# A batch's small state read with token blocks outermost, in a fused attention and two-layer expert kernel

## The chip, the cores and the metric

The kernel runs on one core of one Trainium2 chip. The metric is the device time in microseconds of one execution; lower is better. A number given for a kernel is the median of several executions. One more execution of it was recorded by the hardware profiler, and every duration below is from that record.

## What is computed

Three stages follow each other. The change lies in the attention; the rest is what TensorE spends most of its time on.

```python
# attention, B=4, H=8, S=512 tokens, 32 state rows, D=64
scores  = x @ state.T / sqrt(D);  a  = softmax(scores)   # over the 32 state rows
xread   = a @ state
scores2 = state @ x.T / sqrt(D);  a2 = softmax(scores2)  # over the 512 tokens
sread   = a2 @ x                                         # "read of the state": 32 x 64 a head
# rows of xread and sread, heads side by side: 2176 tokens x 512
h = t @ w_in;  g = h * tanh(softplus(h));  y = g @ w_out # 512 -> 2048 -> 512
# top-1 of 8 experts by the cosine to expert_emb, then
out = gate * (relu(y @ w1[e]) @ w2[e])                   # 512 -> 1024 -> 512
```

All is float32. Large products are made as three products of split operands: each operand is a rounded high part (`WH`, `Ah`, `gh`) and a low rest (`WL`, `Al`, `gl`).

## The kernel before, in words

The engines' programs are written out by hand, one instruction stream for each of TensorE (PE), ScalarE (ACT), VectorE (DVE), GpSimd and the DMA issuer, and they meet at counting semaphores. Nothing is reordered by a scheduler: an instruction that waits holds up all that stands behind it in its engine's stream.

The 2048 hidden columns are taken in 8 pieces of 256 for each batch c (0 to 3), numbered v = 8c + p. For each piece PE computes `H(v)` (line 599: 12 products into PSUM banks 0 and 1, or 6 and 7), ACT and DVE compute the activation together in six passes of 1024 columns (`mish_t`, `mish_w`, `mish_b`, `mish_c`, `mish_hi` on ACT, lines 1032 to 1064; `mish_q`, `mish_e`, `mish_r`, `mish_g`, `mish_lo` on DVE, lines 1500 to 1526), and PE computes `Y(v)` (line 647: 24 products that add to banks 2 to 5). PE's order is H two pieces ahead of Y: H(6), Y(4), H(7), Y(5), H(8), and so on. `H(v)` waits until `mish_q(v-1)` has read its piece out of PSUM, and the first H of a batch c waits for both parts of A, the softmax weights of that batch: `A_hi(c)` on ACT (line 1000, copies `AF` to `Ah`) and `A_lo(c)` on DVE (line 1453, the rest into `Al`).

Beside this runs the attention of the next batch. `M(c, nb)` (line 535) multiplies the state into w_in, and `M_hi` (ACT, line 971) and `M_lo` (DVE, line 1361) take its result out of banks 6 and 7. `score(c)` (line 506) writes banks 6 and 7, `scores_out` (ACT, line 982) takes the scores to `SC`; from batch 1 on it first waits until `SC` was read by the transpose of the batch before (`e2d_rdy`).

The state's read of a batch, `sread(b)` (line 551), is the part that the change is about. `soft_5(b)` (DVE, line 1435) adds 1e-9 to the two sums of each partition, takes their reciprocals, and transposes `SC` into `E2D`. `sread(b)` then makes 128 small products of 32x32 by 32x64: for each of two head groups g and 16 token blocks t, four heads j, each on its own row block and column block of PE's array. The trace has two matmul records and two weight-load records for each of them. For b = 0 all 128 stand between H(6) and Y(4) (line 807); for the others 64 stand at one place and 64 at a later one (`ahead`, `behind`). Before the change b = 0 and 1 run g outermost, with column block j and both groups in bank 6; b = 2 and 3 run t outermost, with column block j^g and bank 6+g. Because column block j^1 puts the heads of group 1 at other partitions, the reciprocals of group 1 are there taken in four instructions of 32 partitions (line 1448). PE waits at `sread(0)` for `e2d_rdy` and for `scores_out(1)` (`sc_e` 4). `sread_scale(b)` (DVE, line 1462) multiplies the result by the reciprocals, `sread_turned(b)` (PE, line 562) transposes it after Y(4), and `sread_out(b)` (ACT, line 1008, four copies for b < 2, or line 1011, two copies) places it in `sh`, which M(1, 0) waits for.

The order around the change is this, u being the piece whose activation is under way. DVE for u = 5: mish_e, mish_r, soft_1(1), mish_g, mish_q(6), mish_lo, sread_scale(0), o_rest(5), soft_sum/soft_3/soft_4(1). DVE for u = 6: mish_e, mish_r, M_lo(1,0), mish_g, mish_q(7), A_lo(1), mish_lo, o_rest(6). ACT for u = 6: mish_b, o_split(6), sread_out(0), mish_t(7), M_hi(1,0), mish_c, mish_w(7), A_hi(1), mish_hi. (`o_split` and `o_rest` split a block of w_out, lines 976 and 1375.)

Of the kernel before, what the change touches and what calls it, by code (L numbers as in the profile page):

```python
# [41 lines left out]
def build(nc, x, state, w_in, w_out, emb, tau, w1, w2, out):  # L42
# [10 lines left out]
    HG = H // 4  # L53
# [30 lines left out]
    def upto(u, e=1):  # L84

        return e + 1 if u == 0 else u + 2
# [26 lines left out]
    with ExitStack() as ctx:  # L113
# [168 lines left out]


        def sr_bank(b, g):
            return 6 if b < 2 else 6 + g

        def sh_upto(b):
            return (4, 8, 10, 12)[b]

        def bv_upto(b):  # L290
            return (2, 4, 10, 16)[b]

        def y_bank(t):
            return 1 if first(t) else 2
# [202 lines left out]
        def _(pe):  # L497
# [41 lines left out]
            def sread(b, part):  # L539
                pe.wait_ge(e2d_rdy, b + 1)  # L540
                if b > 1:
                    pe.wait_ge(m_lo, NB * b + 2)
                elif b == 1:
                    pe.wait_ge(rt_e, ST)
                else:
                    pe.wait_ge(sc_e, 4)
                order = [(g, t) for g in range(HG) for t in range(16)] if b < 2 else [(g, t) for t in range(16) for g in range(HG)]
                for g, t in order[part]:
                    for j in range(4):
                        q = j if b < 2 else j ^ g  # L550
                        mm = pe.matmul(PS[32 * q:32 * q + 32, sr_bank(b, g), D * g:D * g + D], E2D[b][32 * j:32 * j + 32, g, 32 * t:32 * t + 32],  # L551
                                       X2[b % 2][t // 8][32 * j:32 * j + 32, g, t % 8, :],
                                       start=(t == 0), stop=(t == 15))
                if part.stop is None:
                    mm.then_inc(sr_mm, 1)
# [245 lines left out]
            for v in range(B * PC):  # L801
# [3 lines left out]
                if c == 0:  # L805
                    if p == 4:
                        sread(0, whole)
# [123 lines left out]
            with pe.Fori(0, less4) as i:  # L931
                t = (i, 3)
# [16 lines left out]
        def _(act):  # L949
# [16 lines left out]
            def M_hi(c, nb, bank=6):  # L966
                k = NB * c + nb
                act.wait_ge(m_mm, k + 1)
                if k >= NM:
                    act.wait_ge(h_mm, upto(2 * (k - NM) + 1))  # L970
                a.activation(WH[:, k % NM].rearrange("p (g n) -> p g n", g=HG), PS[:, bank:bank + 2, :], ACT.Copy).then_inc(m_hi, 1)

            def o_split(k):
                r = RING["o", k]
                act.wait_ge(in_w[r % NSTAGE], 16 * (r // NSTAGE + 1))
                a.activation(WH[:, 8 + k], raw[:, r % NSTAGE], ACT.Copy).then_inc(o_hi, 1)
# [17 lines left out]
            def A_hi(b, gs=range(HG)):  # L994
                act.wait_ge(af_rdy, HG * b + gs[-1] + 1)
                if b == 1 or b == 2:
                    act.wait_ge(sr_mm, b)
                if b >= 2:
                    act.wait_ge(h_mm, upto((b - 1) * PC - 1))
                a.activation(Ah[:, b % 2, gs[0]:gs[-1] + 1], AF[:, gs[0]:gs[-1] + 1], ACT.Copy).then_inc(a_hi, len(gs))  # L1000

            def sread_out(b):
                act.wait_ge(sh_t, b + 1)
                ps = PS[0:D, 6 if b == 1 else 7, 0:HG * P].rearrange("p (g q r n) -> p g q r n", g=HG, q=2, r=2)
                for h in range(2):
                    if b < 2:
                        for g in range(HG):
                            a.activation(sh[D * h:D * h + D, 2 * g:2 * g + 2, NS * b:NS * b + NS], ps[:, g, :, h if g == 0 else 1 - h, :],
                                         ACT.Copy).then_inc(sh_e, 1)
                    else:  # L1010
                        a.activation(sh[D * h:D * h + D, :, NS * b:NS * b + NS].rearrange("p (g q) n -> p g q n", g=HG), ps[:, :, :, h, :],
                                     ACT.Copy).then_inc(sh_e, 1)
# [42 lines left out]
            def mish_c(u, es=slice(0, 2)):  # L1055
                act.wait_ge(e_rdy, upto(u, es.stop - 1))
                a.activation(ww[:, u % 2, es], ww[:, u % 2, es], ACT.Square, bias=cst[:, 0:1]).then_inc(s_rdy, 1)  # L1057
# [116 lines left out]
            for u in range(1, PC):  # L1174
                mish_b(u)
                if u == 5:
                    scores_out(1)
                if u == 6:
                    o_split(6)
                    sread_out(0)  # L1180
                if u < PC - 1:
                    mish_t(u + 1)
                if u == 2:
                    M_hi(0, 2, 0)
                if u == 3:
                    o_split(3)
                if u == 4:
                    M_hi(0, 3)
                if u == 6:
                    M_hi(1, 0)  # L1190
                mish_c(u)
                if u == PC - 1:
                    o_split(7)
                    break
                mish_w(u + 1)
                if u == 6:
                    A_hi(1)
                mish_hi(u)
                if u == 1:
                    o_split(2)  # L1200
                if u == 3:
                    exp_2(0)
                if u == 4:
                    o_split(4)
                    o_split(5)
                if u == 5:
                    exp_1(1)
# [147 lines left out]
        def _(dve):  # L1355
            v = nc.vector

            def M_lo(c, nb, bank=6):
                k = NB * c + nb
                dve.wait_ge(m_hi, k + 1)  # L1360
                v.tensor_tensor(WL[:, k % NM].rearrange("p (g n) -> p g n", g=HG), PS[:, bank:bank + 2, :],
                                WH[:, k % NM].rearrange("p (g n) -> p g n", g=HG).bitcast(F32), ALU.subtract).then_inc(m_lo, 1)
# [72 lines left out]
            def soft_5(b):  # L1435
                dve.wait_ge(s2_x, 2 * b + 2)
                if b == 1:
                    dve.wait_ge(h_mm, upto(PC - 1))
                v.tensor_scalar(r2[:, b % 2, 2, :], r2[:, b % 2, 2, :], 1e-9, None, ALU.add).then_inc(bv, 1)
                if b < 2:  # L1440
                    dve.wait_ge(bv, bv_upto(b) - 1)
                    v.reciprocal(r2[:, b % 2, 3, :], r2[:, b % 2, 2, :]).then_inc(bv, 1)
                else:
                    dve.wait_ge(bv, bv_upto(b) - 5)
                    v.reciprocal(r2[:, b % 2, 3, 0:1], r2[:, b % 2, 2, 0:1]).then_inc(bv, 1)
                    for j in range(4):
                        q = j ^ 1
                        v.reciprocal(r2[32 * q:32 * q + 32, b % 2, 3, 1:2], r2[32 * j:32 * j + 32, b % 2, 2, 1:2]).then_inc(bv, 1)
                v.transpose(E2D[b][:], SC[:]).then_inc(e2d_rdy, 1)
# [66 lines left out]
            def mish_g(u, es=slice(0, 2)):  # L1516
                dve.wait_ge(qr_rdy, upto(u, es.stop - 1))
                dve.wait_ge(s_rdy, upto(u, es.stop - 1))
                to = qq[:, u % 2, es] if SEQ[u][0] == "m" else gz[SEQ[u][2]][:]
                v.scalar_tensor_tensor(out=to, in0=ww[:, u % 2, es], scalar=0.75, in1=qq[:, u % 2, es],  # L1520
                                       op0=ALU.add, op1=ALU.mult).then_inc(g_rdy, 1)
# [173 lines left out]
            for u in range(1, PC):  # L1695
                mish_e(u)
                mish_r(u)
                if u == 5:
                    soft_1(1)
                if u == 2:  # L1700
                    M_lo(0, 2, 0)
                if u == 4:
                    M_lo(0, 3)
                if u == 6:
                    M_lo(1, 0)
                mish_g(u)
                if u == PC - 1:
                    o_rest(7)
                    break
                mish_q(u + 1)  # L1710
                if u == 6:
                    A_lo(1)
                mish_lo(u)
                if u == 5:
                    sread_scale(0)
                if u == 1:
                    o_rest(2)
                    soft_2(0)
                if u > 2:
                    o_rest(u)  # L1720
                if u == 2:
                    turn_x(1, 0)
                    turn_x(1, 1)
                if u == 3:
                    turn_x(1, 2)
                    turn_x(1, 3)
                if u == 4:
                    soft_5(0)
                if u == 5:
                    soft_sum(1)  # L1730
                    soft_3(1)
                    soft_4(1)
# [231 lines left out]
```

## Time and profile before

| | |
|---|---|
| median of 3 executions | 662.65 us (662.56 to 662.71) |
| profiled execution | 663.51 us, of which the span from first to last instruction is 661.7 us |
| PE busy in the span | 644.3 us, 97% |
| DVE, ACT busy | 441.0 us (67%), 389.7 us (59%) |
| granted TensorE clock | full to within the last 6 us of the span; mean 0.997 |

A view of the trace called the chain of waits follows the work that ended last back to what released each step. The timeline lists instructions of an engine in order of time; "[0.36 <-ACT WH L971]" behind one says that the engine was idle for 0.36 us before it and that line 971 of ACT ended that. "issue" is time in which an engine waited for nothing that the record shows. An instruction may start some 0.1 us before the one before it on its engine has ended.

### The profile page before, as it was taken

The numbers are of one execution on the slowest core, as the hardware profiler recorded it, in microseconds if no ns is written. First come the engines' busy times: TensorE is split into PE (matmuls) and PEld (weight loads), VectorE is DVE, ScalarE is ACT, GpSimd is POOL, SyncE is SP. The second block draws the span as 40 slices with busy tenths as digits, with TensorE's granted clock in tenths as the row PEclk, the third lists the DMA queues.
The fourth block names the chain that finished last, engine by engine and source line by source line (L and its number), as shares of the span: only waits on it lengthen the run. The fifth ranks groups of instructions, "written<-read, shape, count | busy, mean of one in ns | idle before, by whom it ended". The sixth has DMA issues, their size and how long they took to land.

```text
span 661.7 us, 12475 instructions
## 1 busy us (share of the span) xinstructions
PE 644.3 (97%) x4186; PEld 496.8 (75%) x4187; DVE 441.0 (67%) x697; ACT 389.7 (59%) x505; POOL 52.4 (8%) x76
## 2 busy tenths in 40 slices
PE   7899899999999999999999999999999999999996
PEld 5677677677776777776668888788888888888884
DVE  6899999998788689775669668644521631271271
ACT  2898778796668786786877472533421631261260
POOL 2000000000300002100002131100100100100101
PEclk9999999999999999999999999999999999999998
DMA  8913457100533001434000723744511541163140
GB/s 230 273 40 116 174 139 211 64 2 1 152 106 128 1 0 30 166 124 131 0 1 34 263 75 114 274 169 143 191 32 48 175 147 48 48 213 120 48 159 6
DMA packets 35351, 72.73 MB, mean 110 GB/s; under 512 B 5699, under 2 KB 5699, under 8 KB 35312
## 3 DMA queue, kind: packets, MB, share of 16 engines
q1 hardware_dynamic: 27728, 56.93, 26.7%
q0 software_dynamic: 3040, 9.13, 3.5%
q10 hardware_dynamic: 4544, 6.14, 3.0%
q8 instruction: 26, 0.43, 0.3%
q14 instruction: 13, 0.11, 0.1%
HBM read 60.92 MB, written 12.16 MB: 110 GB/s over the span
## 4 chain that ended last, share of the span: by engine, by line
PE 75%; DVE 12%; ACT 6%; issue 3%; DMA 3%; SPq 1%; POOL 0%; ACTq 0%; DVEq 0%; POOLq 0%
PE PS L647 20%; PE PS L754 16%; PE PS L783 16%; PE PS L599 8%; PE PS L763 2%; PE PS L628 2%; PE PS L551 2%; PE PS L535 2%; PE PS L668 1%; DVE ww L1508 1%; ACT ww L1057 1%; DVE qq L1520 1%; PE PS L506 1%; DVE qq L1503 1%; PE PS L735 1%
## 5 line engine op out<-in xcount | busy, mean ns | idle before, releaser
L647 PE MATMUL PS<-WH,gh 128*128 128x512 f32 x256 | 104.0, 406 | 1.4 <-DVE gl L1526 1.3
L647 PE MATMUL PS<-WH,gl 128*128 128x512 f32 x256 | 101.0, 394 | 0.0
L647 PE MATMUL PS<-WL,gh 128*128 128x512 f32 x256 | 100.9, 394 | 0.0
L1157 ACT ACTIVATE hh<-PS 128x512 fp32r<-128x512 f32 x40 | 21.9, 595 | 91.3 <-PE PS L763 88.8
L1602 DVE TENSOR_TENSOR WL<-raw,WH 128x1024 f32 (+1 forms) x48 | 56.0, 1220 | 19.9 <-ACT WH L1137 19.9
L783 PE MATMUL PS<-WH,hh 128*128 (+1 forms) x160 | 65.3, 408 | 0.0
L647 PEld LDWEIGHTS PS<-WH,gh 128*128 128x128 f32 x256 | 48.2, 188 | 19.9 <-issue 6.5
L783 PE MATMUL PS<-WH,hl 128*128 (+1 forms) x160 | 63.1, 394 | 0.0
L783 PE MATMUL PS<-WL,hh 128*128 (+1 forms) x160 | 62.9, 393 | 0.0
L1621 DVE TENSOR_SCALAR osb<-PS,gid 128x512 f32<-128x512 f32 x21 | 15.7, 749 | 66.9 <-PE PS L783 66.9
L1137 ACT ACTIVATE WH<-raw 128x1024 f32 (+1 forms) x48 | 47.6, 1054 | 21.0 <-issue 13.5
L647 PEld LDWEIGHTS PS<-WH,gl 128*128 128x128 f32 x256 | 48.2, 188 | 11.3
L1057 ACT ACTIVATE ww<-ww,cst 128x1024 f32<-128x1024 f32 (+1 forms) x35 | 39.4, 1125 | 28.5 <-DVE ww L1508 28.5
L647 PEld LDWEIGHTS PS<-WL,gh 128*128 128x128 f32 x256 | 48.3, 189 | 10.0
L1503 DVE SCALAR_TENSOR_TENSOR qq<-ww,PS 128x1024 f32<-128x1024 f32 (+1 forms) x35 | 41.4, 1181 | 20.8 <-ACT ww L1045 20.8
L1149 ACT ACTIVATE hsb<-PS 128x512 f32<-128x512 f32 x42 | 24.3, 593 | 51.8 <-PE PS L754 44.3
L1508 DVE SCALAR_TENSOR_TENSOR ww<-ww,rr 128x1024 f32<-128x1024 f32 (+1 forms) x35 | 41.5, 1187 | 15.5 <-ACT rr L1053 15.4
L754 PE MATMUL PS<-WH,yh 128*128 (+1 forms) x168 | 47.7, 405 | 1.3 <-DVE yl L1607 1.3
L754 PE MATMUL PS<-WH,yl 128*128 (+1 forms) x168 | 46.0, 395 | 0.0
L754 PE MATMUL PS<-WL,yh 128*128 (+1 forms) x168 | 45.9, 395 | 0.0
L1607 DVE TENSOR_TENSOR yl<-PS,yh 128x512 fp32r<-128x512 f32 x21 | 14.4, 688 | 47.2 <-ACT yh L1143 47.1
L1520 DVE SCALAR_TENSOR_TENSOR qq<-ww,qq 128x1024 f32<-128x1024 f32 (+1 forms) x33 | 39.3, 1190 | 7.7 <-ACT ww L1057 7.4
(276 smaller groups left out, 1245.9 us busy)
## 6 DMA issues: line engine op xcount, KB each, us to landing
raw<-in_w SPq DMA_DIRECT2D x48, 512.0 KB, 4.6
raw<-in_w_in SPq DMA_DIRECT2D x36, 512.0 KB, 4.9
yg<-by_expert ACTq DMA_DIRECT2D x22, 260.0 KB
raw<-in_w_out SPq DMA_DIRECT2D x8, 512.0 KB, 6.0
by_expert<-junk SPq DMA_DIRECT2D x1, 2080.0 KB, 9.8
wr<-in_w_in SPq DMA_DIRECT2D x4, 512.0 KB, 10.2
x_0a<-in_x SPq DMA_DIRECT2D x8, 128.0 KB, 4.4
x_0b<-in_x SPq DMA_DIRECT2D x8, 128.0 KB, 5.3
```

Source lines behind the costliest of these rows:

```text
L599: mm = pe.matmul(PS[:, h_bank(v) + e, :], w[:, (NB * c + p // 2) % NM, o:o + P], a[:, c % 2, g, :], start=(i == 0 and g == 0), stop=(i == ...
L647: mm = pe.matmul(PS[:, 2 + t, :], a[:, v % 2, e, t * P:t * P + P], w[:, 8 + p, e * 512:e * 512 + 512], start=(p == 0 and e == 0 and i == 0 ...
L754: mm = pe.matmul(PS[:, j, :], a[:, k, :], w[:, bass.ds(slot + k, 1), j * 512:j * 512 + 512].rearrange("p o n -> p (o n)"), start=(i == 0 a ...
L783: mm = pe.matmul(PS[:, o_bank(t, end), :], a[:, m, :], w[:, bass.ds(slot + (KT + m // 2), 1), (m % 2) * 512:(m % 2) * 512 + 512].rearrange ...
L1057: a.activation(ww[:, u % 2, es], ww[:, u % 2, es], ACT.Square, bias=cst[:, 0:1]).then_inc(s_rdy, 1)
L1137: a.activation(WH[:, bass.ds(slot + b, 1), :].rearrange("p o n -> p (o n)"), raw[:, b % NSTAGE], ACT.Copy).then_inc(w_hi, 1)
L1149: a.activation(hsb[:, j * 512:j * 512 + 512], PS[:, j, :], ACT.Relu).then_inc(hs_rdy, 1)
L1157: a.activation(hidden(end)[0][:, 4 * j:4 * j + 4, :], PS[:, 3 + j, :].rearrange("p (k m) -> p k m", k=4), ACT.Copy).then_inc(hh_rdy, 1)
L1503: v.scalar_tensor_tensor(out=qq[:, u % 2, es], in0=ww[:, u % 2, es], scalar=4.0, in1=PS[:, bank + es.start:bank + es.stop, :], op0=ALU.sub ...
L1508: v.scalar_tensor_tensor(out=ww[:, u % 2, es], in0=ww[:, u % 2, es], scalar=4.0, in1=rr[:, es], op0=ALU.add, op1=ALU.mult).then_inc(e_rdy, 1)
L1520: v.scalar_tensor_tensor(out=to, in0=ww[:, u % 2, es], scalar=0.75, in1=qq[:, u % 2, es], op0=ALU.add, op1=ALU.mult).then_inc(g_rdy, 1)
L1602: v.tensor_tensor(WL[:, bass.ds(slot + b, 1), :].rearrange("p o n -> p (o n)"), raw[:, b % NSTAGE], WH[:, bass.ds(slot + b, 1), :].rearran ...
```

## The change

For batch 0 the state's read is done as for batches 2 and 3: t outermost, column block j^g, bank 6+g, reciprocals in five instructions, two copies out. Batch 1 stays as it was. Semaphore counts follow. On ACT `sread_out(0)` moves ahead of `o_split(6)`, and `A_hi(1)` moves from behind `mish_w(7)` to ahead of `mish_c(6)`. On DVE `A_lo(1)` moves from behind `mish_q(7)` to ahead of `mish_g(6)`, and `sread_scale(0)` from behind `mish_lo(5)` to ahead of `mish_q(6)`.

```diff
--- before.py
+++ after.py
@@ -282,13 +282,13 @@
 
 
         def sr_bank(b, g):
-            return 6 if b < 2 else 6 + g
+            return 6 if b == 1 else 6 + g
 
         def sh_upto(b):
-            return (4, 8, 10, 12)[b]
+            return (2, 6, 8, 10)[b]
 
         def bv_upto(b):
-            return (2, 4, 10, 16)[b]
+            return (6, 8, 14, 20)[b]
 
         def y_bank(t):
             return 1 if first(t) else 2
@@ -544,10 +544,10 @@
                     pe.wait_ge(rt_e, ST)
                 else:
                     pe.wait_ge(sc_e, 4)
-                order = [(g, t) for g in range(HG) for t in range(16)] if b < 2 else [(g, t) for t in range(16) for g in range(HG)]
+                order = [(g, t) for g in range(HG) for t in range(16)] if b == 1 else [(g, t) for t in range(16) for g in range(HG)]
                 for g, t in order[part]:
                     for j in range(4):
-                        q = j if b < 2 else j ^ g
+                        q = j if b == 1 else j ^ g
                         mm = pe.matmul(PS[32 * q:32 * q + 32, sr_bank(b, g), D * g:D * g + D], E2D[b][32 * j:32 * j + 32, g, 32 * t:32 * t + 32],
                                        X2[b % 2][t // 8][32 * j:32 * j + 32, g, t % 8, :],
                                        start=(t == 0), stop=(t == 15))
@@ -1003,7 +1003,7 @@
                 act.wait_ge(sh_t, b + 1)
                 ps = PS[0:D, 6 if b == 1 else 7, 0:HG * P].rearrange("p (g q r n) -> p g q r n", g=HG, q=2, r=2)
                 for h in range(2):
-                    if b < 2:
+                    if b == 1:
                         for g in range(HG):
                             a.activation(sh[D * h:D * h + D, 2 * g:2 * g + 2, NS * b:NS * b + NS], ps[:, g, :, h if g == 0 else 1 - h, :],
                                          ACT.Copy).then_inc(sh_e, 1)
@@ -1176,8 +1176,8 @@
                 if u == 5:
                     scores_out(1)
                 if u == 6:
+                    sread_out(0)
                     o_split(6)
-                    sread_out(0)
                 if u < PC - 1:
                     mish_t(u + 1)
                 if u == 2:
@@ -1188,13 +1188,12 @@
                     M_hi(0, 3)
                 if u == 6:
                     M_hi(1, 0)
+                    A_hi(1)
                 mish_c(u)
                 if u == PC - 1:
                     o_split(7)
                     break
                 mish_w(u + 1)
-                if u == 6:
-                    A_hi(1)
                 mish_hi(u)
                 if u == 1:
                     o_split(2)
@@ -1437,7 +1436,7 @@
                 if b == 1:
                     dve.wait_ge(h_mm, upto(PC - 1))
                 v.tensor_scalar(r2[:, b % 2, 2, :], r2[:, b % 2, 2, :], 1e-9, None, ALU.add).then_inc(bv, 1)
-                if b < 2:
+                if b == 1:
                     dve.wait_ge(bv, bv_upto(b) - 1)
                     v.reciprocal(r2[:, b % 2, 3, :], r2[:, b % 2, 2, :]).then_inc(bv, 1)
                 else:
@@ -1703,16 +1702,15 @@
                     M_lo(0, 3)
                 if u == 6:
                     M_lo(1, 0)
+                    A_lo(1)
                 mish_g(u)
                 if u == PC - 1:
                     o_rest(7)
                     break
-                mish_q(u + 1)
-                if u == 6:
-                    A_lo(1)
-                mish_lo(u)
                 if u == 5:
                     sread_scale(0)
+                mish_q(u + 1)
+                mish_lo(u)
                 if u == 1:
                     o_rest(2)
                     soft_2(0)
```

## Rows read from the trace of the kernel before

**Rows 1.** The page: the chain that ended last, by engine.

```profile
PE 75%; DVE 12%; ACT 6%; issue 3%; DMA 3%; SPq 1%; POOL 0%; ACTq 0%; DVEq 0%; POOLq 0%
```

**Rows 2.** The chain of waits, 60 to 100 us: start us, us, what.

```profile
75.67 3.48 PE PS L551 x238
79.15 1.70 issue
80.85 0.52 PE PS L551 x18
...
90.12 1.02 PE PS L535 x16
...
96.92 0.11 issue
```

**Rows 3.** Timeline of DVE: start us, us, engine, line, operation, operands, count [idle before].

```profile
72.44 0.16 DVE L1439 TENSOR_SCALAR r<-r 128x2 f32<-128x2 f32 x1
...
72.71 1.23 DVE L1449 STREAM_TRANSPOSE E2D<-SC 128x1024 f32<-128x1024 f32 x1
74.18 1.23 DVE L1508 SCALAR_TENSOR_TENSOR ww<-ww,rr 128x1024 f32<-128x1024 f32 x1 [0.24 <-ACT rr L1053]
...
128.24 1.22 DVE L1449 STREAM_TRANSPOSE E2D<-SC 128x1024 f32<-128x1024 f32 x1
129.39 1.18 DVE L1508 SCALAR_TENSOR_TENSOR ww<-ww,rr 128x1024 f32<-128x1024 f32 x1
...
166.91 0.16 DVE L1439 TENSOR_SCALAR r<-r 128x2 f32<-128x2 f32 x1
...
168.04 1.25 DVE L1449 STREAM_TRANSPOSE E2D<-SC 128x1024 f32<-128x1024 f32 x1
```

**Rows 4.** Timeline of ACT, around the scores of batches 1 and 2.

```profile
74.05 1.03 ACT L982 ACTIVATE SC<-PS 128x1024 f32<-128x1024 f32 x1
75.71 1.02 ACT L1041 ACTIVATE ww<-PS 128x1024 f32<-128x1024 f32 x1 [0.63 <-PE PS L599]
...
129.58 1.03 ACT L982 ACTIVATE SC<-PS 128x1024 f32<-128x1024 f32 x1 [2.48 <-DVE E2D L1449]
```

**Rows 5.** Timeline of PE, halves of sread(1) and of sread(2).

```profile
159.58 1.10 PE L551 MATMUL PS<-x_1a,E2D 32*32 32x64 f32 x64
160.50 1.07 PE L551 MATMUL PS<-x_1b,E2D 32*32 32x64 f32 x64
...
186.35 1.48 PE L551 MATMUL PS<-x_0a,E2D 32*32 32x64 f32 x128
```

**Rows 6.** DMA queues, 78.3 to 79.3 us: packets, MB, share of 16 engines.

```profile
q8 instruction: 1, 0.02, 5.5%
```

**Rows 7.** Windows: us, busy (and instructions) of PE, PEld, DVE, ACT, POOL, clock, DMA share, GB/s.

```profile
77.25:80.85 3.60, 1.90 (x137) 1.74 (x125) 3.46 (x4) 1.47 (x2) 0.00 (x0) 1.00 0.02 5
80.90:101.80 20.90, 20.79 (x128) 14.79 (x129) 20.10 (x22) 15.18 (x19) 0.00 (x0) 1.00 0.53 138
```

**Rows 8.** Timeline of DVE, 80 to 98 us.

```profile
80.20 1.22 DVE L1520 SCALAR_TENSOR_TENSOR qq<-ww,qq 128x1024 f32<-128x1024 f32 x1
...
83.68 0.47 DVE L1462 TENSOR_SCALAR shn<-PS,r 128x64 f32<-128x64 f32 x2
...
90.73 1.22 DVE L1513 SCALAR_TENSOR_TENSOR qq<-qq,rr 128x1024 f32<-128x1024 f32 x1
92.31 1.23 DVE L1361 TENSOR_TENSOR WL<-PS,WH 128x1024 fp32r<-128x1024 f32 x1 [0.36 <-ACT WH L971]
...
94.58 1.21 DVE L1503 SCALAR_TENSOR_TENSOR qq<-ww,PS 128x1024 f32<-128x1024 f32 x1
95.71 1.22 DVE L1453 TENSOR_TENSOR Al<-AF,Ah 128x1024 fp32r<-128x1024 f32 x1
```

**Rows 9.** Timeline of ACT, 90 to 97 us.

```profile
91.25 1.03 ACT L971 ACTIVATE WH<-PS 128x1024 fp32r<-128x1024 f32 x1
...
94.16 1.05 ACT L1000 ACTIVATE Ah<-AF 128x1024 fp32r<-128x1024 f32 x1
```

## Prediction

> **What bounds the kernel now.** I read the page's chain first: three quarters of it is PE [rows 1], so time taken off PE, or off what PE waits for, should show. Then the chain of waits around the changed read [rows 2]. The reader is to see two holes in PE. One is 1.70 us long and lies inside `sread(0)`, after 238 of its 256 matmul records; it ends for nothing the record shows. The other is 0.11 us at 96.92, just before H(8). Everything between them is PE work back to back. So the changed read costs PE 81.37 − 75.67 = 5.7 us, of which 4.0 are work.
>
> Last come the timelines of DVE and ACT, since PE at H(8) depends on them. DVE is nearly without a gap from `mish_e(5)` at 74.18, which follows a gap of 0.24 us, to `mish_r(6)` at 90.73; then it waits 0.36 us for `M_hi(1,0)`, and runs `M_lo(1,0)`, `mish_g(6)`, `mish_q(7)` and `A_lo(1)` back to back [rows 3, 8]. `A_lo(1)` ends at 95.71 + 1.22 = 96.93, and H(8), which needs it, starts at 97.03. So two chains end at H(8) almost together: PE's own (Y(5) ends at 96.92) and DVE's. A gain needs both to be shorter.
>
> **PE's part: the matmuls.** The rows have both orders. Half of sread(1), g outermost, lasts from 159.58 to 161.57, 1.99 us; half of sread(2), t outermost, 1.48 us [rows 5]. Between starts that is about 15 ns a record against 11 ns, so the whole read would shrink by 2 × 0.51 = 1.0 us, if nothing else held it.
>
> **PE's part: the hole.** What it is decides what is left of that. A packet of 16 KB (the 0.02 MB of its row) on an instruction queue lies in 78.3 to 79.3 us, the only DMA there (5.5% of 16 engines for 1 us is 0.88 us) [rows 6]. PE resumes at 80.85. From 77.25 to 80.85 the trace has 137 + 125 = 262 PE records, and from 80.90 to 101.80, a stretch nearly six times as long, it has 128 + 129 = 257 [rows 7]. I take it that each packet is a block of some 256 instructions, asked for when PE enters a block, and that the block after the present one is needed before 3.6 us have passed (77.25 to 80.85). Then the hole's end hangs on when PE was at about its 110th matmul record of `sread(0)`, not on how fast the rest goes. A faster read uses the block up earlier and waits longer: only the first 110 records (110 × 4 ns = 0.4 us) and the last 18 (0.1 to 0.2 us, being spread over 0.52 us in the rows) are gained, together 0.55.
>
> The Trainium skill ("Runtime: NRT & Kernel Launch", section "Instruction fetch mechanics") says that code comes in blocks of 16 KiB, fetched ahead while the present one runs, with 2048 instructions held for PE, and that the cost is mostly hidden. By that rule the hole would be something else and the read would gain its full 1.0 us. The packet's size agrees; the 1.70 us hole beside a packet speaks against "hidden". I take the fetch-bound value.
>
> **PE's part: a later start.** `soft_5(0)` gets five reciprocals for one. Before, 72.71 − 72.44 = 0.27 us pass from its first instruction to the transpose; in batch 2, which has the new form, 168.04 − 166.91 = 1.13 [rows 3]. The transpose thus starts 0.86 later, at 73.57. `scores_out(1)` on ACT waits for it: with 129.58 − 128.24 = 1.34 from transpose start to ACT start [rows 3, 4] it begins at 74.91, not 74.05, and ends at 75.94. `sread(0)` waits for these scores and so starts at 76.0, not 75.67: 0.35 us lost. H(6) is done by then, so nothing covers it. `mish_t(6)` had 0.63 us of idle time before it and moves by some 0.15 only [rows 4]. PE's sum: +0.35 − 0.55 = −0.2 us at Y(4).
>
> **DVE's part.** `mish_e(5)` follows the transpose by 1.15 (128.24 to 129.39) [rows 3], so it starts at 74.72 instead of 74.18: +0.54. What follows is in order and gapless, so the lag travels. `sread_scale(0)` costs the same at its new place (0.39 us to the next start) if the read is over by then: it comes behind `mish_g(5)`, at 80.20 + 0.54 + 1.13 = 81.87, and the read ends at about 81.2, so 0.6 us are left. One wait goes with the move: `mish_lo(5)` no longer stands right behind `mish_q(6)` after waiting for `mish_hi(5)`, −0.09 (from `mish_g(5)` to `sread_scale(0)` are three starts in 83.68 − 80.20 = 3.48 us, where 95.71 − 94.58 = 1.13 each would make 3.39 [rows 8]; the range has 0). Lag at `mish_r(6)`: +0.45. There DVE had its gap: it could have started the next instruction at 90.73 + 1.13 = 91.86 and started it at 92.31, so 0.45 is there to take it. So `M_lo(1,0)` starts at 92.3, as before, now bound by DVE instead of by ACT [rows 8].
>
> **The moves of A.** After `M_lo(1,0)` DVE has the same four instructions before H(8) can start, in another order. `A_hi(1)` takes the place behind `M_hi(1,0)`: 92.2 to 93.2 instead of 94.16; `A_lo(1)` can start at 93.45. `mish_c(6)` ends at 94.3, `mish_g(6)` starts at 94.58; `mish_w(7)` ends at 95.2, `mish_q(7)` starts at 95.71 and ends at 96.92 [rows 8, 9]. H(8) also waits for `mish_q(7)`, since that frees its banks. So the last of the four ends at 96.9 as before, only it is another one: the wait for `A_lo(1)` becomes a wait for `mish_q(7)`. `mish_hi(6)` and `mish_lo(6)` start as before. `sread_out(0)` and `o_split(6)` swap inside an ACT gap before `mish_t(7)`; two copies fewer save ACT 0.2 us there, hidden. No DMA issue or wait of the SP queue moves by more than the 0.5 us of `o_rest(5)`; its load is wanted at M(1,1), near 100 us. If that cover were gone, M(1,1) would wait by up to 0.5.
>
> **Sum.** PE is 0.2 us ahead at Y(4), loses this at H(8), and H(8) starts at 97.03 + 0.0. Behind it no order is changed. The profiled execution took 663.51 us, so 663.5 again; the median of before lies 0.86 lower, which gives 662.7. Bounds: PE and DVE could both be ahead at H(8) if the reciprocals cost less than in batch 2, down to −0.45 (the gap of DVE), and −1.0 if DVE's waits fell otherwise too; upwards +0.54 if no gap takes the lag, and +1.0 by the third rival.
>
> **The rivals.**
> First, *the matmuls' gain reaches the end* (faster). It needs the hole to be free of the fetch, and DVE to be ahead too. PE's sum is then +0.35 − 1.0 = −0.65, or −2.35 with the hole gone: 662.0 or 660.3 us. For it: the rates of rows 5. Against: DVE's slack of 0.45 before `M_lo(1,0)` is eaten by the reciprocals. The skill's rule on hidden fetches, cited above, belongs to this rival. 0.10.
> Second, *the new quadrants give no speed* (the change does not do what it says, for instance because two groups of one block still load their weights one after another): 15 ns a record. Then the block is entered 0.4 later, the hole ends at 81.25, Y(4) and M(1,0), which ended at 91.14 [rows 2], come 0.35 later, and with them M_hi, M_lo and H(8): 663.0 us. Against it: batches 2 and 3 have this form at 11 ns. 0.08.
> Third, *DVE queues behind the read* (slower). `sread_scale(0)` now stands ahead of `mish_q(6)`; from the point at which the read ends after 81.8, each microsecond goes onto DVE and from there onto H(8). Say the code fetch takes as much longer as the hole is long, 1.7 us: the read ends at 82.9, the lag is 1.0 more, 663.7 us. For it: the place is in the code, and the margin is only 0.6 us. Against: nothing makes the fetch slower. 0.12.
> Fourth, *the lag isn't absorbed*: 0.54 us of DVE time show in full: 663.2 us. 0.08.
>
> **Numbers.** The forecast has 0.62. About 0.2% (1.3 us) is what a measurement can tell from no change; the forecast, the second and fourth rival and most of the third stay within it, as does half of the first. So same 0.90, faster 0.05, slower 0.05. The range of 8 in 10 takes in the forecast, the second and fourth rival, the milder half of the first and the third nearly to its price: 661.9 to 663.6 us.
>
> **What would show it.** `sread(0)` starts near 76.0, with a hole of 2 us or more ending near 80.9; the transpose into `E2D` starts near 73.6; no idle time on DVE before `M_lo(1,0)` near 92.3; a wait for `mish_q(7)` at H(8), near 97.0. I am wrong if the hole shrinks or is gone, if DVE is idle for long before `sread_scale(0)`, or if H(8) starts more than 0.5 us from 97.03.

## The result and the profile after

The changed kernel takes 664.52 us (median of 17 executions, 663.32 to 665.96); the kernel before, run beside it, 663.01 (17 executions, 662.56 to 664.18). The ratio is 1.0021, 95% interval 1.0014 to 1.0028: slower by 1.5 us, just past the 0.2% (1.3 us) that the prediction takes for no change, and outside its range. The profiled execution took 664.86 us. The page:

```profile
span 663.1 us, 12477 instructions
...
PE 69%; DVE 16%; ACT 7%; issue 4%; DMA 2%; ACTq 0%; SPq 0%; POOL 0%; DVEq 0%; POOLq 0%
```

PE's share of the chain fell from 75% [rows 1] to 69%. The chain of waits around the read (start us, us, what) answers to [rows 2]:

```profile
75.77 2.51 PE PS L551 x146
78.28 1.91 issue
80.19 0.41 PE PS L551 x18
80.59 7.32 PE PS L647 x24
...
90.89 1.10 PE PS L535 x16
...
92.02 1.04 ACT WH L971
...
93.08 0.97 DVE WL L1360
...
96.57 1.14 DVE qq L1502
...
97.75 3.02 PE PS L599 x12
```

The read's 238 records take 2.51 us instead of 3.48 (the chain counts only 146 of them; PE's timeline lists all 238 ahead of the hole), the hole is 1.91 instead of 1.70 and starts after the same 238 records, and then comes what the prediction has nowhere: Y(4), the 24 matmuls of line 647, takes 7.32 us. Before, it took 5.79 (from 81.36). The windows (columns as in [rows 7]) show why:

```profile
78.28:80.19 1.91, 0.00 (x2) 0.01 (x1) 1.81 (x2) 0.24 (x1) 0.00 (x0) 1.00 0.00 0
81.00:84.00 3.00, 3.00 (x9) 2.35 (x8) 3.00 (x5) 2.37 (x3) 0.00 (x0) 0.50 0.02 5
84.50:87.50 3.00, 3.00 (x14) 2.44 (x13) 2.83 (x5) 1.24 (x2) 0.00 (x0) 1.00 0.28 83
```

In the hole PE does nothing. A stretch of granted clock 0.50 follows it, 3.41 us long in this execution (80.82 to 84.24), in which 9 matmuls fit into 3 us where 14 do at full clock: 1.2 instead of 2.4 GHz. Y(4) loses 1.5 us by it. DVE's timeline answers to [rows 3, 8]:

```profile
72.10 0.16 DVE L1438 TENSOR_SCALAR r<-r 128x2 f32<-128x2 f32 x1
...
73.23 1.25 DVE L1448 STREAM_TRANSPOSE E2D<-SC 128x1024 f32<-128x1024 f32 x1
...
81.51 0.47 DVE L1461 TENSOR_SCALAR shn<-PS,r 128x64 f32<-128x64 f32 x2
81.90 1.21 DVE L1502 SCALAR_TENSOR_TENSOR qq<-ww,PS 128x1024 f32<-128x1024 f32 x1
...
93.08 1.23 DVE L1360 TENSOR_TENSOR WL<-PS,WH 128x1024 fp32r<-128x1024 f32 x1 [1.04 <-ACT WH L971]
```

DVE now waits 1.04 us before `M_lo(1,0)`, since PE is late, not 0.36. Measured from `soft_5(0)`'s first instruction, H(8) starts at 97.75 − 72.10 = 25.65 us; before it was 97.03 − 72.44 = 24.59: 1.06 of the 1.4 us by which the spans differ. Up to `soft_5(0)` the changed profile is 0.34 us shorter and from H(8) to the end 0.63 longer. Most of this last part lies in the routing, far behind the change. PE's timelines, before and then changed, have PE's return from a wait near 332 us and from another near 426 us:

```profile
332.10 0.73 PE L599 MATMUL PS<-Ah,WH 128*128 128x512 f32 x2 [1.29 <-DVE qq L1503]
425.70 1.20 PE L754 MATMUL PS<-WH,yh 128*128 x4 [1.29 <-DVE yl L1607]
```

```profile
333.00 0.73 PE L599 MATMUL PS<-Ah,WH 128*128 128x512 f32 x2 [1.28 <-DVE qq L1502]
427.06 1.19 PE L754 MATMUL PS<-WH,yh 128*128 x4 [1.54 <-DVE yl L1606]
```

From the one to the other are 93.60 us before and 94.06 after. In all six profiles with the new read (changed, e1, e2, e6, e7, e9) it is 93.83 to 94.06, in the eight without it 93.56 to 93.63. In the same six a load of a table entry on ACT (TENSOR_LOAD), some 8 us before PE's return, takes 0.44 to 0.64 us instead of 0.28. ACT has two instructions fewer in them, the two copies saved, but no run tried that by itself, so the cause stays open. So 0.25 to 0.45 us belong to the change and come from behind H(8).

The 17 mean clocks and times go together: 663.3 to 663.8 us at 0.998 and 0.999, 664.4 to 665.1 at 0.996 and 0.997, 665.7 to 666.0 at 0.993 to 0.995. One stretch of 3.41 us at half clock lowers the mean by 0.0026.

### The profile page after: what moved, and what is told of

Read it like the earlier page. It is cut to its first block, busy times and chain, and to the rows that moved or that the text cites. A ratio compares the mean times of both kernels' runs of the same rounds, so it can differ in the third digit from the quotient of the medians.

```text
span 663.1 us, 12477 instructions
## 1 busy us (share of the span) xinstructions
PE 644.2 (97%) x4186; PEld 496.6 (75%) x4187; DVE 441.7 (67%) x701; ACT 389.9 (59%) x503; POOL 52.3 (8%) x76
## 4 chain that ended last, share of the span: by engine, by line
PE 69%; DVE 16%; ACT 7%; issue 4%; DMA 2%; ACTq 0%; SPq 0%; POOL 0%; DVEq 0%; POOLq 0%
PE PS L647 17%; PE PS L754 16%; PE PS L783 16%; PE PS L599 7%; PE PS L763 2%; DVE qq L1519 2%; PE PS L628 2%; PE PS L551 2%; DVE ww L1507 2%; DVE qq L1502 2%; PE PS L535 2%; ACT ww L1057 2%; PE PS L668 1%; DVE gl L1525 1%; PE PS L735 1%
## 5 line engine op out<-in xcount | busy, mean ns | idle before, releaser
L1157 ACT ACTIVATE hh<-PS 128x512 fp32r<-128x512 f32 x40 | 21.9, 596 | 91.7 <-PE PS L763 89.2
```

What stands on the lines that cost most here:

```text
L1157: a.activation(hidden(end)[0][:, 4 * j:4 * j + 4, :], PS[:, 3 + j, :].rearrange("p (k m) -> p k m", k=4), ACT.Copy).then_inc(hh_rdy, 1)
```

## The experiments

Three theories were set against each other. Theory 1: an idle stretch of PE, here the hole, makes the granted clock fall. Theory 2: the denser read itself, on eight blocks of the array instead of four, does it (the expectations below say 16, which was a slip). Theory 3: the cost is DVE's (reciprocals, moves). The table has, for one profiled execution each, the longest idle time of PE between the read's start and H(8), and the starts of `M_lo(1,0)` and H(8) after `soft_5(0)`'s first instruction; for all executions the median and how many had a mean clock of 0.996 or less (the half clock in the last 1 to 4 us of the span is in that mean too, so this counts roughly: a mean of 0.997 can hide one stretch of 3.41 us, as in the profile of e5, and a mean of 0.998 or more can't).

| kernel | idle, us | M_lo(1,0) | H(8) | median, us | low clock |
|---|---|---|---|---|---|
| before | 1.70 | +19.87 | +24.59 | 663.01 to 663.47 in four sessions | 8 of 78 |
| changed | 1.91 | +20.98 | +25.65 | 664.52 | 9 of 17 |
| e2_read_only | 2.09 | +19.94 | +24.66 | 664.51 | 3 of 11 |
| e3_moves_only | 1.31 | +19.45 | +24.13 | 663.18 | 2 of 11 |
| e1_split_new | 2.40 | +20.00 | +24.67 | 665.18 | 6 of 12 |
| e4_split_old | 1.35 | +19.43 | +24.15 | 663.00 | 0 of 11 |
| e9_split_new_dense | 0.68 | +20.02 | +24.69 | 663.83 | 1 of 12 |
| e10_longer_pocket | 2.60 | +20.71 | +25.42 | 665.88 | 4 of 7 |
| e11_split_old_moves | 2.42 | +20.55 | +25.22 | 664.52 | 5 of 12 |

**e1_split_new: the new read without its hole.**

```diff
                 if c == 0:
                     if p == 4:
-                        sread(0, whole)
+                        sread(0, ahead)
+                        Y(v, (0,))
+                        sread(0, behind)
...
-                Y(v, (1,) if v == 0 or c in (1, 2)
+                Y(v, (1,) if v in (0, 4) or c in (1, 2)
```

> The changed kernel with the read of batch 0 in two halves, 64 products before Y(4) and 64 after its first 12 matmuls. Theory 1 (the 1.91 us hole in the read lets the granted clock fall to half in Y(4), and the hole is a wait for a code block): no hole over 0.5 us in the read, no stretch of half clock before the end of PE's work, Y(4)'s 24 matmuls in 5.6 us of PE time, time at or up to 0.6 us below the kernel before (662.4 to 663.1), and runs close together. Theory 2 (the denser pattern on 16 array blocks pulls the clock down by itself): half clock appears in Y(4) all the same, 664 to 665. Theory 3 (the lag of DVE from four more reciprocals and the moves cost it): clock full, but 663.5 to 664.5.

It took 665.18 us (663.51 to 667.92; ratio 1.0023, 1.0008 to 1.0038). PE's timeline, then windows:

```profile
75.82 1.47 PE L551 MATMUL PS<-x_0a,E2D 32*32 32x64 f32 x128 [0.44 <-ACT SC L984]
...
96.83 1.06 PE L599 MATMUL PS<-Ah,WH 128*128 128x512 f32 x2 [2.40 <-DVE qq L1504]
```

```profile
94.30:96.80 2.50, 0.13 (x1) 0.00 (x0) 2.50 (x4) 1.13 (x2) 0.00 (x0) 1.00 1.06 227
97.20:100.20 3.00, 3.00 (x8) 2.30 (x7) 3.00 (x4) 1.63 (x2) 0.00 (x0) 0.50 0.34 75
```

Half of the read is one dense run of 1.47 us, the hole is gone, Y(4) runs at full clock. But PE is now so early that it waits 2.40 us for DVE before H(8), and the half clock is there instead, behind that idle stretch. Theory 1 in its narrow form (the hole) failed and so did its time; what stayed is an idle stretch in either place, or theory 2.

**e2_read_only and e3_moves_only: the change in two.** e2 is the changed kernel with `A_hi(1)`, `A_lo(1)`, `sread_scale(0)` and `sread_out(0)` put back; e3 is the kernel before with only these four moved.

```diff
--- changed
+++ e2_read_only (ACT, then DVE)
-                    sread_out(0)
                     o_split(6)
+                    sread_out(0)
...
-                    A_hi(1)
                 mish_c(u)
...
                 mish_w(u + 1)
+                if u == 6:
+                    A_hi(1)
...
-                    A_lo(1)
                 mish_g(u)
...
-                if u == 5:
-                    sread_scale(0)
                 mish_q(u + 1)
+                if u == 6:
+                    A_lo(1)
                 mish_lo(u)
+                if u == 5:
+                    sread_scale(0)
```

> The changed kernel with all four moves undone (A's two parts, the scale, the copies out back at their old places); the new read and its reciprocals stay. Theory 1: hole of about 1.9 us and half clock in many executions as in the changed kernel, 663.8 to 665. Theory 3 with the moves as the cause: back to 663.0. If the moves helped at all, it is slower than the changed kernel by up to 0.5 us, since the scale of the read on DVE comes later and A's low part last.

> The kernel before with the four moves alone; the read stays g outermost. Theories 1 and 2: read, hole (1.7 us) and full clock as before, H(8) at the same distance behind the read, time within 0.3 us of before (662.8 to 663.3). Theory 3 with the moves as the cause: 664 or more.

e2 took 664.51 us (ratio 1.0021, 1.0012 to 1.0030), e3 663.18 (1.0000, 0.9991 to 1.0008). As far as the medians tell, the whole loss is the read's, with its reciprocals; the moves cost nothing and, in the changed kernel, gain nothing. Not all of e2's slow executions show a low clock: of six at 664.5 us and above, three have a mean of 0.996 or less, two 0.997 and one 0.998; e1 has one of 665.19 us at 0.999. So part of the spread has another cause, which stays open. The profiled execution of e2 kept its clock:

```profile
80.38 0.41 PE L551 MATMUL PS<-x_0b,E2D 32*32 32x64 f32 x18 [2.09 <-issue]
...
96.77 0.48 PE L599 MATMUL PS<-Ah,WH 128*128 128x512 f32 x1 [0.42 <-issue]
```

```profile
81.00:84.00 3.00, 3.00 (x14) 2.42 (x14) 3.00 (x4) 2.36 (x3) 0.00 (x0) 1.00 0.02 5
```

So a 2.09 us hole does not always cost the clock, and this execution shows the rest of the change alone: H(8) at +24.66. DVE's timeline of e3, with the old read:

```profile
72.78 0.16 DVE L1438 TENSOR_SCALAR r<-r 128x2 f32<-128x2 f32 x1
...
92.23 1.22 DVE L1360 TENSOR_TENSOR WL<-PS,WH 128x1024 fp32r<-128x1024 f32 x1
```

`M_lo(1,0)` starts at 92.23 − 72.78 = 19.45, with DVE gapless before it. The hole of e3 was 1.31 us. DVE's gap of 0.36 us in [rows 8] belonged to an execution with a long hole.

**e4_split_old: the old read in halves**, the edit of e1 on the kernel before.

> The kernel before with its own order of the read, but in two halves around Y(4)'s first 12 matmuls. If the hole is the wait for a code block: it is gone or under 0.5 us, the read and Y(4) end 1.2 to 1.7 us earlier, and of this DVE lets 0.3 to 0.5 us through at H(8): 662.5 to 662.8. If the hole has another cause tied to the place (a wait on some engine), it stays and the time is 663.0.

663.00 us, against 663.47 beside it; ratio 0.9998 (0.9989 to 1.0007), no difference. PE's timeline:

```profile
80.08 1.09 PE L551 MATMUL PS<-x_0a,E2D 32*32 32x64 f32 x64
81.00 1.07 PE L551 MATMUL PS<-x_0b,E2D 32*32 32x64 f32 x64
...
96.19 0.70 PE L599 MATMUL PS<-Ah,WH 128*128 128x512 f32 x2 [1.35 <-issue]
```

The hole is gone, as expected, and PE stands idle 1.35 us before H(8) instead, in front of DVE's chain. H(8) comes at +24.15, as in e3: PE's time is worth nothing here.

**e6_shift: is the hole a wait for code?** The changed kernel with

```diff
-            keep_warm(20)
+            keep_warm(28)
```

> The changed kernel with 8 more dummy products at PE's start: 16 more matmul and 16 more weight-load records, 60 us ahead of the read. If the hole is the wait for a code block of a fixed number of instructions, it moves 16 matmul records forward, to behind the 222nd of 256, and keeps its end at some 3 to 3.6 us behind the entry into the block. If it belongs to the place in the read or to another engine, it stays behind the 238th.

The chain of waits:

```profile
76.41 2.38 PE PS L551 x138
78.79 2.09 issue
80.88 0.84 PE PS L551 x34
```

Behind the hole stand 34 records instead of 18: it came after the 222nd. It has moved by exactly the 16 records added 65 us earlier, which no wait on another engine would do. Half clock is granted from 80.91 us on, as the hole ends. A second, smaller hole (0.7 us) turned up in a later read, and the one execution took 666.46 us.

**e12_t_outer_same_columns: what makes the read faster.** In the kernel before, t outermost and bank 6+g, but q = j kept.

```diff
-            return 6 if b < 2 else 6 + g
+            return 6 if b == 1 else 6 + g
...
-                order = [(g, t) for g in range(HG) for t in range(16)] if b < 2 else [(g, t) for t in range(16) for g in range(HG)]
+                order = [(g, t) for g in range(HG) for t in range(16)] if b == 1 else [(g, t) for t in range(16) for g in range(HG)]
```

> The kernel before with token blocks outermost and a bank for each head group, but each head still on its own row and column block (no exclusive or), so both groups use the same four array blocks. If the other column blocks give the speed: 14 to 15 ns a matmul record as before. If the order or the banks give it: 11 ns. The hole stays behind the 238th record, and is 1.3 to 2.1 us long.

```profile
75.31 1.99 PE L551 MATMUL PS<-x_0a,E2D 32*32 32x64 f32 x128
...
79.89 0.52 PE L551 MATMUL PS<-x_0b,E2D 32*32 32x64 f32 x18 [1.04 <-issue]
```

128 records take 1.99 us, as before (15 ns each): order and banks give nothing. The speed comes from the other column blocks (`j^g`), and with them come the split reciprocals. The hole was only 1.04 us long with the same rate, so its length differs between executions. 662.77 us (one execution).

**e8_recips_only: the reciprocals' price.** The kernel before with `soft_5(0)` in five reciprocals (and the counts of `bv_upto` to suit).

```diff
-                if b < 2:
+                if b == 1:
                     dve.wait_ge(bv, bv_upto(b) - 1)
...
-                        q = j ^ 1
+                        q = j if b == 0 else j ^ 1
```

> The kernel before with five reciprocals instead of one for batch 0, and nothing else. Transpose into E2D 0.86 us later behind soft_5's first instruction, the read 0.35 us later, DVE's gap before M_lo(1,0) (0.36 us) gone, H(8) at most 0.2 us later as seen from soft_5's first instruction; time unchanged within noise.

```profile
72.89 0.16 DVE L1439 TENSOR_SCALAR r<-r 128x2 f32<-128x2 f32 x1
...
73.89 1.25 DVE L1449 STREAM_TRANSPOSE E2D<-SC 128x1024 f32<-128x1024 f32 x1
...
92.69 1.22 DVE L1361 TENSOR_TENSOR WL<-PS,WH 128x1024 fp32r<-128x1024 f32 x1
```

Here the transpose comes at +1.00, not +1.13 (against 0.27), and `M_lo(1,0)` at +19.80 without a gap, H(8) at +24.52. Seen from the profile of before H(8) is unchanged, as expected; seen from e3, e4 and e12 (+24.13 to +24.15) it is 0.4 later.

**e7_split_new_filled and e9_split_new_dense: filling the idle stretch.** Ahead of H(8) in e1, 9 dummy products of 128 columns (e7), or 2 of 512 (e9):

```diff
+                if v == 6:
+                    pe.wait_ge(m_lo, NB + 1)
+                    for _ in range(2):
+                        pe.matmul(PS[:, 7, :], ident[:], stBD[:, 0].rearrange("p c n -> p (c n)"), start=True, stop=True)
                 if v + 2 < B * PC:
                     H(v + 2)
```

> e1_split_new (new read in two halves) with 9 dummy products, about 2 us of dense PE work into bank 7, before H(8), where PE had stood idle for 2.4 us. Theory 1, now widened (any pocket in which PE has nothing dense to do can cost the full clock, wherever it lies): the pocket is under 0.6 us, the executions at 665 and above go, 11 of 12 lie within 663.2 to 664.2, median 663.5. Theory 2 (the denser pattern pulls the clock down): the spread of e1_split_new stays, median 664.5 to 665.5. Filling gives no time back beyond that, since DVE sets H(8).

e7 did not do what was expected: 664.74 us (663.94 to 668.17, 8 executions; ratio 1.0038, 1.0024 to 1.0053). PE's idle time before H(8) was down to 0.37 us in its profile, and 2 of the 8 had a low mean clock. But three of its executions took 664.5 to 664.9 at a mean clock of 0.999, so that was not the clock. Its 36 added instructions also move all later code blocks, as e6's 32 did; between the routing matmuls at 156 and 388 us its profile is 0.5 us longer than e1's. That this is the cause was not tried by itself, which is why e9 followed.

> e1_split_new with two dummy products of 512 columns (4 matmul records, about 1.7 us of dense work, 8 instructions) in PE's pocket before H(8). Unlike the 9 small ones of e7_split_new_filled they move the code blocks behind them by 8 instructions only. Pocket theory (an idle stretch of PE of some 2 us and more is what costs the full clock): pocket under 0.9 us, at most 2 executions in 11 above 664.7, median 663.3 to 663.9. Pattern theory (the read on 16 array blocks costs the clock wherever it stands): half of the executions above 664.7 as in e1_split_new.

```profile
96.76 0.73 PE L599 MATMUL PS<-Ah,WH 128*128 128x512 f32 x2 [0.68 <-DVE qq L1508]
```

663.83 us (663.39 to 665.15; ratio 1.0011, 1.0003 to 1.0020), with H(8) where it was in e1 (+24.69). The only edit to e1 is dummy work, and it takes 1.35 us off the median; measured against the kernel before of its own session each, e1 is 1.7 us above it and e9 0.8, so 0.9 us are the safer figure. With the idle stretch short, the 0.8 us that are left fit the DVE lag of 0.5 and the 0.25 to 0.45 lost in the routing.

**e10_longer_pocket and e11_split_old_moves: the old read with a long idle stretch.** e10 is e4 with the transpose behind A made twice on DVE; e11 is e4 with the four moves (the edits of e1 and of e2 reversed). e10, in `soft_4`:

```diff
+                if b == 1:
+                    av_link(v.transpose(AF[:], PT[:]))
+                    av_join()
```

> e4_split_old (old pattern of the read, in halves) with the transpose that makes A of batch 1 done twice on DVE: 1.2 us more in the chain that H(8) waits for, so PE's pocket before H(8) grows from 1.4 to some 2.6 us. DVE's chain alone: H(8) 1.2 us later, and that less a slack of up to 0.6 at the end: 663.6 to 664.3 with the executions close together. Pocket theory: besides, a third or more of the executions 1.5 us and more above the fastest, as in e1_split_new, and mean clocks of 0.996 and less among them. Pattern theory: no such executions, since the read is the old one.

```profile
97.43 0.69 PE L599 MATMUL PS<-Ah,WH 128*128 128x512 f32 x2 [2.60 <-issue]
```

```profile
98.20:101.20 3.00, 3.00 (x8) 2.32 (x8) 3.00 (x4) 0.52 (x2) 0.00 (x0) 0.50 0.27 72
```

e10 took 665.88 us (7 executions; ratio 1.0032, 1.0019 to 1.0045): three at 664.5 to 664.8 with a clock of 0.998, four at 665.9 to 666.4 with 0.995 and 0.996. Of e10's distance to e4, 1.27 us is the added transpose itself, by which H(8) comes later; the split into two groups with different clocks is what bears on the theories. The read has the old pattern, so theory 2 falls.

> The kernel before with the read in halves (old pattern) and the four moves: no hole, no added reciprocals, the scale before mish_q(6) without a wait if the second half ends in time. If DVE's chain sets H(8): 24.0 to 24.2 us behind soft_5's first instruction as in e3_moves_only and e4_split_old, time 662.6 to 663.2, so the two don't add up. If they add up: 0.8 us below before.

Both of its expectations were wrong: 664.52 us (ratio 1.0020, 1.0010 to 1.0031). DVE's timeline:

```profile
83.05 0.47 DVE L1463 TENSOR_SCALAR shn<-PS,r 128x64 f32<-128x64 f32 x2 [1.12 <-PE PS L551]
```

The second half of the read ends only at 83 us, and `sread_scale(0)` at its new place waits for it, with `mish_q(6)` and the rest of DVE's chain behind it: H(8) 1.1 us later than in e4, an idle stretch of 2.42 us, and 3.41 us of half clock from 98.02 us on, 0.14 us before the stretch ends. This is the third rival's mechanism, made by an experiment; in the changed kernel the read ended in time and nothing waited.

**e5_later_g: can H(8) come earlier?** e4 with `mish_g(6)` behind `A_lo(1)` and `mish_q(7)`, `o_rest(6)` ahead of `mish_lo(6)`, and `A_hi(1)` and `mish_w(7)` ahead of `mish_c(6)`.

```diff
                 if u == 6:
                     M_lo(1, 0)
+                    A_lo(1)
+                    mish_q(u + 1)
                 mish_g(u)
...
-                mish_q(u + 1)
                 if u == 6:
-                    A_lo(1)
+                    o_rest(u)
+                else:
+                    mish_q(u + 1)
                 mish_lo(u)
```

> The kernel before with its own order of the read in two halves (as e4_split_old), and DVE's four instructions before H(8) cut to three: A's low part and mish_q(7) come first, mish_g(6) behind them, o_rest(6) ahead of mish_lo(6); on ACT A's high part and mish_w(7) ahead of mish_c(6). If DVE's chain is what holds H(8): H(8) starts 1.0 to 1.2 us earlier than in e4_split_old, seen from the E2D transpose, the idle pocket of PE before it shrinks from 1.4 to under 0.5 us, and 0.3 to 1.1 us reach the end: 661.9 to 662.7. If it is not: pocket and time as in e4_split_old (663.0), or slower because mish_lo(6) is late for Y(6).

H(8) came at +22.95, 1.20 us earlier than in e4: DVE's chain is what holds it. The time was 663.37 us (ratio 1.0003, 0.9994 to 1.0012). The routing matmul at 156 us stood at +83.35 against +82.81 in e4, and on the way there PE waited for `mish_q` again, 1.18 us at 106 and 0.27 us at 118, where e4 has no such wait. What is gained at H(8) is lost before 156 us.

The profiled execution of e5 also has a stretch of half clock far from the read, and it follows a shorter idle stretch than in any other profile:

```profile
23.15 1.19 PE L613 MATMUL PS<-Ah,WL 128*128 128x512 f32 x2 [1.22 <-DVE WL L1371]
```

```profile
23.25:26.55 3.30, 3.30 (x8) 2.47 (x9) 2.67 (x5) 2.40 (x3) 0.00 (x0) 0.50 1.08 192
```

Its mean clock was 0.997, so the count in the table misses it. In the fourteen profiles together PE stands idle for 1.9 us or more six times (changed, e1, e2, e6, e10, e11) and for 1.0 to 1.8 us 61 times; half clock is granted in or right behind five of the six, and behind one of the 61.

No version beat the kernel before by more than its measurement is uncertain.

## Why the prediction was wrong

**What held.** The read starts 0.5 us later after `soft_5(0)` begins (75.77 − 72.10 = 3.67 against 75.60 − 72.44 = 3.16; forecast 0.35). It runs at 11 ns a record, its hole lengthens and comes after the same 238 records, and Y(4) starts at +8.49 against +8.92, 0.43 us earlier where 0.2 was forecast. The hole is a wait for code: e6 shows it, and the rival by which the gain reaches the end is refuted. The Trainium skill ("Runtime: NRT & Kernel Launch", section "Instruction fetch mechanics") calls this cost mostly hidden; here it was 1.0 to 2.1 us for 512 instructions in a row. H(8) ended up waiting for `mish_q(7)`, as said. In the profile of e2, which kept its clock, the time saved on PE was lost at H(8), as said.

**The step that failed: "PE is 0.2 us ahead at Y(4), loses this at H(8)".** It took idle time of PE as free. The sum has nothing for the stretch from the end of the hole to H(8), and gives no reason; it was 1.5 us in the profiled execution, since the clock was halved for 3.41 us. H(8) came at +25.65 instead of +24.59, beyond the 0.5 us that the prediction names as a sign of being wrong, and DVE stood idle for 1.04 us before `M_lo(1,0)`, where it expected none. The hole itself was foreseen ("2 us or more"), the fall behind it was not; the granted clock was full in the profile of before, with a hole of 1.70 us, and I read this as safety. e10 and e11 (old read, idle 2.60 and 2.42 us, half clock behind it), e1 (idle moved, half clock moved with it) and e9 (idle filled, low mean clock in 1 of 12 executions instead of 6 of 12) show that an idle stretch of PE is what can cost the clock, wherever it lies. It happens in some executions of the same kernel, which is why e2's profile lacks it. That the hole of the changed kernel itself does it rests on the order of events in two profiles (changed and e6: half clock from 80.8 and 80.9 us, within 1 us of the hole's end) and on the counts: 12 of 28 executions with the new read and its hole, 8 of 78 before.

**The term that was mis-sized: DVE's slack of 0.45 us.** "0.45 is there to take it" was read from one execution. Its hole was 1.70 us long; with 1.31 (e3), 1.04 (e12) or none (e4) DVE has no gap and `M_lo(1,0)` starts at +19.43 to +19.45. With the new read and full clock it starts at +19.94 to +20.02. The lag of 0.5 us is thus paid in most executions, as far as these profiles can stand for the rest; the fourth rival, given 0.08, was right in kind. The sum took 0.86 us off for the median execution and kept the slack of the slower, profiled one.

**A second term of nothing: "Behind it no order is changed".** Between 332 and 426 us the new read loses 0.25 to 0.45 us, in six profiles of six; the prediction calls the two copies saved on ACT hidden and has no term there. With the lag of 0.5 us this fits the lowest times, 663.32 after and 662.56 before, which differ by 0.76. The starting point was low as well: 662.65 us from three executions, 663.01 from the 17 beside the changed kernel, 0.36 of the 1.8 us by which the forecast of 662.7 is off.

**The sum as it stands.** About 0.5 us of DVE lag and 0.25 us or more in the routing in nearly every execution, and 0.8 to 2.4 us more in 11 of the 17 (664.4 to 666.0 against 663.6), by the clock as far as the mean clocks show it. The median is one of the 11.

The Trainium skill ("TensorE: Matmul & The Clock Gate", section "HAM oscillation — how this bites in real kernels") describes PE waiting between bursts of work and starting the next at the lower clock. The waits that the Trainium skill has there are 3 to 5 us long and come in each pass of a loop. The traces here agree in kind, with single and shorter waits of 1.9 to 2.6 us (once 1.22) in an otherwise full PE, and not each time (e2, 2.09 us).

## What to carry to other kernels

Where PE is faster than the engine that feeds it, a saving on PE becomes an idle stretch, and the idle stretch may cost more than the saving by the clock behind it. Leave such a stretch short; filling it with dense work of few instructions took back part of the loss here (e9), and with many small products it took back nothing (e7). A gap on another engine that is to absorb added work has to be seen in several executions, since it can be the shadow of a wait whose length varies. Long runs of very short matmuls can use up code faster than it arrives (here 512 instructions at 5 to 7 ns each); put longer matmuls between them, and expect every instruction added on PE to move such holes elsewhere.

## What the runs showed of the hardware that was not expected

- An idle stretch of PE of 1.9 to 2.6 us was followed in some executions by half clock for 3.41 us (the changed kernel, e1, e6, e10, e11). With at most 1.35 us between read and H(8) (e4) 0 of 11 executions had a low mean clock. A short stretch is no guarantee: 1.22 us at 21.9 us were followed by it in the profile of e5, the only one of 61 between 1.0 and 1.8 us.
- 16 + 16 added records at PE's start moved a hole 65 us later by exactly 16 matmul records (e6).
- Products on 32x32 blocks run at 15 ns a record on four blocks and 11 ns on eight; order and PSUM banks made no difference (e12).
- With the new read, whose result leaves in two instructions fewer on ACT, PE needs 93.83 to 94.06 us instead of 93.56 to 93.63 from its return near 332 us to that near 426 us (six profiles against eight); the cause is open.
